# Attention's result reaches the first MLP with the head dimension on partitions, by DMA shifts instead of turns on TensorE

## The reference

```python
# attention: q, k, v are (2, 8, 1152, 64)
q_pool = q.reshape(B, H, S // 2, 2, D).mean(axis=3)              # 576 queries per head
scores = q_pool @ k.T / sqrt(D);  attn = exp(scores - max)
attn = attn / (sum(attn) + 1e-9);  out = attn @ v
x = out.transpose(0, 2, 1, 3).reshape(1152, 512)                 # tokens x (head, head dim)
# first MLP: 512 -> 2048 -> 512
h = x @ w_in;  g = P(h) / (Q(h) + 1e-6);  x = g @ w_out          # P cubic, Q quadratic in |h|
# second MLP: 512 -> 1536 -> 512
xn = x / rms(x) * rms_g;  out = (silu(xn @ w_gate) * (xn @ w_val)) @ w_out2
```

## Time and profile before

| what | value |
|---|---|
| runs of the kernel | 698.08, 700.30 and 1152.23 us; median 700.3 us |
| the profiled execution, by its own time | 701.52 us |
| its span in the trace | 699.7 us |
| PE, PEld (weight loads), DVE, ACT, POOL busy | 98%, 92%, 75%, 60%, 60% of the span |
| attention, first MLP, second MLP | to about 252, to about 457, to the end |

### The profile page before, as it was taken

The page is one execution under the profiler, slowest core; times in us unless marked ns, Lnnn a source line. Parts: engine busy times, 40 slices in busy tenths (PEclk is TensorE's granted clock), DMA queues, the critical chain, the costliest instruction groups (busy, mean ns, idle before and its releaser), DMA issues.

```text
span 699.7 us, 12101 instructions
## 1 busy us (share of the span) xinstructions
PE 686.1 (98%) x4039; PEld 640.5 (92%) x4039; DVE 528.0 (75%) x1026; ACT 420.6 (60%) x874; POOL 417.7 (60%) x417
## 2 busy tenths in 40 slices
PE   8999999999999998899999999999999999999998
PEld 6899999999999998799999998889999999999996
DVE  6889999999999988878898888987654444444432
ACT  5778878888887879777788888954411111111110
POOL 6788878778787576978798788864534430000000
PEclk9999999999999999899999999999999999999999
DMA  8684444634442030101101110113210300000012
GB/s 235 232 216 129 132 132 141 183 114 139 131 122 52 4 119 1 60 1 61 60 17 45 61 61 2 60 61 98 85 60 9 113 1 0 1 1 1 0 61 75
DMA packets 21916, 53.79 MB, mean 77 GB/s; under 512 B 2672, under 2 KB 4784, under 8 KB 21744
## 3 DMA queue, kind: packets, MB, share of 16 engines
q1 hardware_dynamic: 21584, 52.90, 24.5%
q10 hardware_dynamic: 288, 0.33, 0.2%
HBM read 41.42 MB, written 2.36 MB: 63 GB/s over the span
## 4 chain that ended last, share of the span: by engine, by line
PE 87%; POOL 5%; DMA 3%; ACT 2%; issue 1%; SPq 1%; DVE 1%; POOLq 0%; DVEq 0%; ACTq 0%
PE hb L781 30%; PE ob L824 24%; PE sc L667 10%; PE sc L675 8%; PE pv_ps L693 5%; PE misc L693 4%; PE tb L781 3%; DMA qrawA<-in_q 2%; DMA km_lo<-kqB 1%; PE misc L714 1%; POOL num L628 1%; POOL wi_lo L582 1%; PE tb L775 1%; POOL num L626 1%; POOL kqB L520 0%
## 5 line engine op out<-in xcount | busy, mean ns | idle before, releaser
L1069 DVE TENSOR_REDUCE neg_part<-sc 128x1 f32<-128x384 f32 x216 | 108.1, 551 | 12.1 <-PE sc L667 9.9
L894 ACT ACTIVATE pt_hi<-sc 128x384 fp32r<-128x384 f32 x216 | 90.5, 493 | 44.3 <-PE sc L675 44.3
L1080 DVE TENSOR_TENSOR pt_lo<-sc,pt_hi 128x384 fp32r<-128x384 f32 x216 | 106.6, 549 | 2.4 <-ACT pt_hi L894 2.1
L824 PE MATMUL ob<-wo_hi,gt_hi 128*128 128x512 f32 x252 | 100.9, 400 | 4.8 <-DVE gt_lo L1173 2.8
L824 PE MATMUL ob<-wo_lo,gt_hi 128*128 128x512 f32 x252 | 100.6, 399 | 0.0
L824 PE MATMUL ob<-wo_hi,gt_lo 128*128 128x512 f32 x252 | 100.4, 399 | 0.0
L781 PE MATMUL hb<-xt_hi,wi_hi 128*128 128x384 f32 x280 | 95.6, 341 | 0.0
L781 PE MATMUL hb<-xt_lo,wi_hi 128*128 128x384 f32 x280 | 94.4, 337 | 0.0
L781 PE MATMUL hb<-xt_hi,wi_lo 128*128 128x384 f32 x280 | 94.4, 337 | 0.0
L885 ACT ACTIVATE prob<-sc,neg_max 128x1152 f32<-128x1152 f32 x72 | 89.2, 1239 | 3.1 <-DVE neg_max L1073 3.1
L675 PE MATMUL sc<-ident,prob 128*128 128x128 f32 x648 | 82.6, 273 | 0.2 <-ACT prob L885 0.2
(11 more groups left out here) (169 smaller groups left out, 1730.1 us busy)
## 6 DMA issues: line engine op xcount, KB each, us to landing
wraw<-in_moe_w_out SPq DMA_DIRECT2D x7, 1024.0 KB, 5.0
krawB<-in_k SPq DMA_DIRECT2D x8, 576.0 KB, 3.9
qrawB<-in_q SPq DMA_DIRECT2D x8, 512.0 KB, 4.9
wraw<-in_moe_w_in SPq DMA_DIRECT2D x4, 1024.0 KB, 5.2
krawA<-in_k SPq DMA_DIRECT2D x7, 576.0 KB, 5.2
qrawA<-in_q SPq DMA_DIRECT2D x7, 512.0 KB, 6.0
wraw<-in_moe_w_gate SPq DMA_DIRECT2D x3, 1024.0 KB, 4.9
...
```

The costliest lines, as they stand in the source:

```text
L824: ins = nc.tensor.matmul(ob[(m + 1) % 2][:], gt[i][:, f, P * t:P * t + P], wo[c % 2][j][:, f, :], start=f == 0 and n == 0, stop=f == CHUNK ...
L894: nc.scalar.activation(pt[0][:, 3 * c:3 * c + 3, PT_COL[i]:PT_COL[i] + P], src, ACT.Copy).then_inc(pt_hi, 1)
L1069: nc.vector.tensor_reduce(neg_part[:, s, c:c + 1], sc[s][:, c, 0:KBANK], AX.X, ALU.max, negate=True).then_inc(part_done, 1)
L1080: nc.vector.tensor_tensor(pt[1][:, kt, col], src, pt[0][:, kt, col].bitcast(F32), ALU.subtract).then_inc(pt_lo, 1)
```

## The change

`combine`, `divide`, `rows_copy`, `gather`, the turns of tokens for the first MLP and the buffers `o_rows` are gone. Instead SP copies the two halves of `o_sb` to the partitions that the head has in the MLP's input (`shift`, two DMAs inside SBUF), and turns the reciprocals of the row sums into a row that stands on 64 partitions (`rows_of_recip`: DMA to DRAM number by number, a wait, a DMA back that is broadcast). In every second pair POOL sums the halves, scales them and splits them for two heads at once (`sum_parts`, `scale_rows`, `split_x`, 1152 columns each). The last pair goes in pieces: POOL does the columns of groups 0 and 1 (`last_x`), between the splits of the first and the second weights; DVE and ACT do groups 2 and 3 during the first units (`last_scaled`, `last_hi`, `last_lo`). Unit 0 waits for POOL's pieces (`x_lo`); group 3's products stand behind unit 0. `xt` is kept from the start; the buffer `wraw` of raw weights shares its place with attention's, so the first weights are loaded in the last pair. In pair 0 group 0's products move ahead of a scores product, and POOL splits the values ahead of the low queries. POOL's loop over pairs is written out.

```diff
+HALF = KEYS // 2
+
+SUMMED = (0, 5, TILES)
...
+        xt = [sbuf(top, f"xt_{x}", [P, DK, TOKENS], F32R) for x in ("hi", "lo")]
...
-        wraw = sbuf(top, "wraw", [P, DK, CHUNK * P])
...
+            def shift(h, par, n):
+
+                if par == 0:
+                    sp.wait_ge(x_lo, n + 1)
+                sp.wait_ge(o_evac, h * 4 + 4)
+                for e in range(2):
+                    sp.dma_start(o_part[e][64 * par:64 * par + 64, :], o_sb[64 * e:64 * e + 64, :]).then_inc(shifted, 16)
+
+            def rows_of_recip(h, par):
+
+                sp.wait_ge(recip_done, h * 2 + 2)
+                with nc.allow_non_contiguous_dma(reason="one number of each row for each of nine tiles"):
+                    sp.dma_start(recip_rows[par].rearrange("t p -> p t"), recip[:, par]).then_inc(row_out, 16)
+                sp.wait_ge(row_out, h * 16 + 16)
+                sp.dma_start(r_row[64 * par:64 * par + 64, :],
+                             recip_rows[par].rearrange("t p -> (t p)").partition_broadcast(64)).then_inc(row_in, 16)
+
+            def last_rows(n):
+
+                t0, t1 = SUMMED[n], SUMMED[n + 1]
+                sp.wait_ge(recip_done, 2 * PAIRS + 2 * n)
+                with nc.allow_non_contiguous_dma(reason="one number of each row for some tiles"):
+                    sp.dma_start(recip_rows[1, t0:t1].rearrange("t p -> p t"), recip[:, 1, t0:t1]).then_inc(tail_out[n], 16)
+                sp.wait_ge(tail_out[n], 16)
+                sp.dma_start(r_row[64:128, P * t0:P * t1],
+                             recip_rows[1, t0:t1].rearrange("t p -> (t p)").partition_broadcast(64)).then_inc(tail_row[n], 16)
+
+            def last_shift(g):
+
+                sp.wait_ge(o_evac, 4 * PAIRS - 3 + g)
+                col = group_cols(g)
+                for e in range(2 if g < 2 else 1):
+                    sp.dma_start(o_part[e][64:128, col], o_sb[64 * e:64 * e + 64, col]).then_inc(tail_in[g], 16)
+
+            def pair(h, par, n):
+
+                if is_last(h):
+                    mixed_keys(1, h)
+                    load_w(sp, *order[0])
+                    shift(h - 1, 1 - par, n)
+                    rows_of_recip(h - 1, 1 - par)
+                    last_shift(0)
+                    last_rows(0)
+                    last_shift(1)
+                    sp.wait_ge(w_split, 8)
+                    load_w(sp, *order[1])
+                    last_rows(1)
+                    last_shift(2)
+                    last_shift(3)
+                    return
...
-                for x in range(2):
-                    sp.wait_ge(v_split[x], h * 2 + 2)
-                    load_v(x, h + 1)
+                sp.wait_ge(v_split[0], h * 2 + 2)
+                load_v(0, h + 1)
+                if is_first(h):
...
+                else:
+                    shift(h - 1, 1 - par, n)
+                sp.wait_ge(v_split[1], h * 2 + 2)
+                load_v(1, h + 1)
+                if not is_first(h):
+                    rows_of_recip(h - 1, 1 - par)
                 mixed_keys(0, h + 1)
...
+            def sum_parts(h, n):
+
+                pool.wait_ge(k_split[0], h * 2)
+                pool.wait_ge(shifted, n * 64 + 64)
+                nc.gpsimd.tensor_tensor(o_part[0][:], o_part[0][:], o_part[1][:], ALU.add).then_inc(x_sum, 1)
+
+            def scale_rows(n):
+
+                pool.wait_ge(x_sum, n + 1)
+                pool.wait_ge(row_in, n * 32 + 32)
+                nc.gpsimd.tensor_tensor(o_part[0][:], o_part[0][:], r_row[:], ALU.mult).then_inc(x_scaled, 1)
+
+            def split_x(n):
+
+                nc.gpsimd.tensor_scalar(xt[0][:, n], o_part[0][:], 1.0, 0.0, ALU.mult, ALU.add).then_inc(x_hi, 1)
+                pool.wait_ge(x_hi, n + 1)
+                nc.gpsimd.tensor_tensor(xt[1][:, n], o_part[0][:], xt[0][:, n].bitcast(F32), ALU.subtract).then_inc(x_lo, 1)
+
+            def last_x(part, col, n):
+
+                y, d = o_part[0][part, col], DK - 1
+                nc.gpsimd.tensor_tensor(y, y, o_part[1][part, col], ALU.add).then_inc(x_sum, 1)
+                pool.wait_ge(x_sum, n)
+                nc.gpsimd.tensor_tensor(y, y, r_row[part, col], ALU.mult).then_inc(x_scaled, 1)
+                pool.wait_ge(x_scaled, n)
+                nc.gpsimd.tensor_scalar(xt[0][part, d, col], y, 1.0, 0.0, ALU.mult, ALU.add).then_inc(x_hi, 1)
+                pool.wait_ge(x_hi, n)
+                nc.gpsimd.tensor_tensor(xt[1][part, d, col], y, xt[0][part, d, col].bitcast(F32), ALU.subtract).then_inc(x_lo, 1)
+
...
+                if n is not None:
+                    scale_rows(n)
+                    pool.wait_ge(x_scaled, n + 1)
                 mixed_sum(h)
-            def divide(h, par, late):
-
...
-                rows = o_rows[:, 0:TILES - 1]
-                nc.gpsimd.tensor_tensor(rows[:, :, 0:HEAD_DIM], rows[:, :, 0:HEAD_DIM], rows[:, :, HEAD_DIM:], ALU.add).then_inc(rows_sum, 1)
-                pool.wait_ge(rows_sum, h + 1)
-                nc.gpsimd.tensor_tensor(tok[:, :, bass.ds(h * HEAD_DIM, HEAD_DIM)], o_rows[:, :, 0:HEAD_DIM],
-                                        recip[:, par].unsqueeze(2).to_broadcast([P, TILES, HEAD_DIM]), ALU.mult).then_inc(rows_done, 1)
+                if n is not None:
+                    split_x(n)
 
...
-            def pair(h, par):
+            def pair(h, par, n):
                 if is_last(h):
                     pool.wait_ge(k_split[1], h * 2 + 2)
                     values_free(1, h)
                     values_hi(1)
                     values_lo(1, h)
-                    divide(h - 1, 1 - par, False)
-                    for x in range(2):
-                        for f in range(CHUNK):
-                            split_w(order[x], f)
+                    for f in range(CHUNK):
+                        split_w(order[0], f)
+                    pool.wait_ge(w_split, 8)
+                    pool.wait_ge(shifted, 32 * h)
+                    pool.wait_ge(row_in, 16 * h)
+                    last_x(slice(0, 64), slice(HALF, TOKENS), n + 1)
+                    pool.wait_ge(tail_row[0], 16)
+                    for g in range(2):
+                        pool.wait_ge(x_lo, n + 2 + g)
+                        pool.wait_ge(tail_in[g], 32)
+                        last_x(slice(0, P), group_cols(g), n + 2 + g)
+                    for f in range(CHUNK):
+                        split_w(order[1], f)
                 else:
                     split_first_half(h + 1)
-                    if not is_first(h):
-                        divide(h - 1, 1 - par, True)
-                    split_second_half(h + 1)
+                    batch = par == 0 and not is_first(h)
+                    if batch:
+                        sum_parts(h + 1, n)
+                    split_second_half(h + 1, n if batch else None)
 
...
-            def combine(h, part, par):
-
...
-                for n, t in enumerate(PARTS[part]):
-                    ins = nc.tensor.transpose(part_bank(part, par, is_last(h))[:, P * n:P * n + P], o_sb[:, P * t:P * t + P], ident[:])
-                ins.then_inc(comb_t, 1)
-
...
-                    elif i >= 4 or not is_first(h):
+                    elif is_first(h) and i <= 4:
+                        if i >= 3:
+                            pv(0, h, *((0, 8) if i == 3 else (8, 2 * KEY_TILES)))
+                    else:
                         g, j0, j1 = PV_AT[i]
                         pv(g, h, j0, j1)
-                    if i == 2 and not is_first(h):
-                        combine(h - 1, 0, 1 - par)
-                        combine(h - 1, 2, 1 - par)
-                    if i == 3 and not is_first(h):
-                        combine(h - 1, 1, 1 - par)
-                    if i == 7 and is_last(h):
-                        combine(h, 0, par)
-                    if i == 8 and is_last(h):
-                        for t in range(4):
-                            turn_tokens(t, False)
...
-                if f == 0 and c in (0, NC1):
-                    pe.wait_ge(xt_lo, (TILES if mlp2 else 0) + BT * nb + BT)
+                if f == 0 and c == 0:
+                    if nb == 0:
+                        pe.wait_ge(x_lo, PAIRS // 2 + 3)
+                        pe.wait_ge(pt_lo, 27 * PAIRS - 3)
+                    else:
+                        pe.wait_ge(tail_lo, nb)
+                if f == 0 and mlp2 and c == NC1:
...
-            pv(3, PAIRS - 1, 0, 2 * KEY_TILES)
             for u in range(UNITS * NC1):
                 first_product(u)
                 if u == 0:
-                    combine(PAIRS - 1, 1, 1)
-                    combine(PAIRS - 1, 2, 1)
-                for t in TURNED_AT.get(u, ()):
-                    turn_tokens(t, False)
+                    pv(3, PAIRS - 1, 0, 2 * KEY_TILES)
...
-                    act.wait_ge(comb_t, h * 3)
-                nc.scalar.activation(o_sb[:, o0:o0 + n], pv_bank(g, is_last(h) and g == 3)[:, 0:n], ACT.Copy).then_inc(o_evac, 1)
-
...
+            def last_hi(g):
```

(33 more changed lines are left out.)

318 lines of the change are left out of this document (122 added, 196 removed).

## The result

The changed kernel takes 725.0 us (median of four runs, 723.4 to 725.3), the kernel before 699.7 beside it: a ratio of 1.0365 [1.0337, 1.0393]. (One of the four executions of the kernel before took 1152.23 us; the ratio is taken without it.) It is slower by 3.7%, 22 us above the forecast of 703 and outside its range. The profiled run took 725.3, its span is 723.5; the first unit of the MLP stands at 273.25, where the forecast had 253.0.

The account below looks back on a forecast made before the run. PE bounds each pair, POOL with ACT the MLP's first units. None of eleven us of removed PE work arrives; span 699.7 + 2.7 = 702.4, 704.2 against the profiled run, 703 against the median; range 696 to 709.

Parts of the forecast that it names:

- I take 4: SP's queue, each pair: the scatter of 1152 numbers to DRAM takes 4 us, bounds 2.5 and 5.6.
- Behind the scatter's wait stands the copy of the keys `km`, wanted a pair later: nothing: SP's queue in attention: the keys' copy queued behind the scatter's wait costs no time.
- Rival 3: Last pair: SP's two scatters delay POOL's rows once they and SP's issues exceed 12.7 us; 708 us up, chance 0.08.
- Its case of three times the row: Last pair's scatters: writing a 4-byte piece costs three times the reading row, 26.1 us, giving 716 us or more.
- Attention's turns: PE in attention: removing nine turns of `o_sb` from each of seven pairs saves 0.6 us a pair, bounds 0.3 and 0.89.
- The start: First pairs: weights' load leaves the first 20 us, value matmuls fill idle PE, `km_lo` wait goes; gain 1.3 us, bounds 0 and 1.8.
- PE's waits for `v2A` in pairs 3 and 5: First value matmuls of pairs 3, 5 and 7: PE waits 1.53 us because POOL's scaling stands ahead of the values.
- POOL's dependent row as the bound of the first unit: Last pair into MLP: POOL's dependent steps take 35.6 us, first unit starts at 253.0, after a 7.1 us PE wait.
- a clock of 0.50 behind the wait: PE at the MLP's first unit: after about 7 us idle it returns at half speed, 3.84 instead of 1.92 us.
- Pair 3 at 30.23: PE in attention: pairs 3 and 5 near 30.2 us, from 1.53 us of waiting less 0.89 of removed turns.
- The ramp's: MLP's first units: a 5.1 us later start shrinks to a 2.7 us shift at unit 4, which stays; bounds 0 and 5.5.
- The signs named ahead: Trace signs of a wrong forecast: first-unit wait under 3 us or due to a DMA, scatter over 6 us, all pairs alike.

Follow-up runs that it names:

- e4: Changed kernel plus separately waited-for DMA probes in the first MLP; probe g wrote 512 4-byte pieces (7.8 us), another all 1152 (10.9 us); run 756.2 us.
- e9: Changed kernel with each scatter of 4-byte pieces replaced by five serial, waited-for writes of 36-byte runs; 716.1 us, ratio 1.0221 to the kernel before.
- e1: Changed kernel without any scatters or SP's waits for them, rows read from a row of the weights; 700.56 us, ratio 1.0018 to the kernel before.

## Why the prediction was wrong

**The step that failed** is "I take 4" for the scatter of 1152 numbers, with its bounds of 2.5 and 5.6, and with it "Behind the scatter's wait stands the copy of the keys `km`, wanted a pair later: nothing". SP stood 9.0 us at the scatter in its place and 10.9 alone. The bounds came from the one row of 4-byte pieces in the earlier trace rows, but that was a read: 512 pieces from DRAM in 2.5 us. As many written cost 7.8 alone (e4, g). Direction was taken to be of no weight, and both bounds rested on that; the true price lay at 1.6 to 1.9 times the upper one. Nor was `km` wanted a pair later: the copy issued at 130.30 was wanted at 137.85, in the third tile step of the next pair. Rival 3 had the right place, the right chain and the right threshold (12.7 us for two scatters): from the shift at 237.62 to the second broadcast at 263.70 SP took 26.1 us, 13.4 more than that, and POOL's row ended 12.3 late. Its case of three times the row, 26.1 us and 716 us, was closest, yet it stood at a chance of 0.08 because the range of the row was trusted.

**What even rival 3 did not have** is attention. It counts SP's wait in the last pair alone, but SP stands about as long in every pair from 1 on, and behind the wait the copies of `km` go out in one bunch with the broadcast and the next loads. Those of `km_lo` took 7.3 us where they had taken 3.1, and in pairs 4 and 6 PE stood 3.04 and 2.30 us for them, where the prediction had nothing. By e9 the bunch alone makes them late. In pair 4 the copy came 2.3 us later than in e9; 0.9 of that is the longer stand, and where the other 1.4 come from no run shows.

**The sum, step by step.** The first unit came 20.25 us late (273.25 against 253.0): pair 7 began 7.9 late (225.31 against 217.4), and POOL needed 47.9 us from there instead of 35.6, 12.3 more: the two waits for `r_row` are 14.4, and the rest of its row was 2.1 shorter than forecast. Behind the first unit it took 450.2 us, 0.8 more than the forecast's 449.4. Of the 7.9, 5.3 are the waits for `km_lo`. Without scatters (e1) the first two nearly vanish: 218.39, and 34.2 from there.

**Attention's turns** were mis-sized: 0.3 us a pair arrived, not 0.6, the lower bound. DVE shows why, at the maxima of pair 2:

```profile
70.11 1.49 DVE L1109 TENSOR_REDUCE neg_part<-sc 128x1 f32<-128x384 f32 x3 [0.28 <-PE sc L752]
...
89.25 1.49 DVE L1109 TENSOR_REDUCE neg_part<-sc 128x1 f32<-128x384 f32 x3 [0.29 <-PE sc L752]
```

Behind 70.11 DVE's timeline shows no wait until 89.25: through tiles 0 to 4 it is DVE that sets the pace, and the turns stood in tiles 2 and 3. PE had slack there and gets none of it back.

**The start** came nearly as forecast, but not in pair 0. PE's timeline before, then after:

```profile
41.54 1.14 PE L675 MATMUL sc<-ident,prob 128*128 128x128 f32 x9
...
72.06 1.14 PE L675 MATMUL sc<-ident,prob 128*128 128x128 f32 x9
```

```profile
41.43 1.14 PE L760 MATMUL sc<-ident,prob 128*128 128x128 f32 x9
```

Pair 1 begins only 0.1 us earlier. But the wait for `km_lo` of the earlier trace rows, at 50.61, lies in pair 1 and is gone: that pair took 30.52 us and now 70.61 - 41.43 = 29.18, 1.34 less, of which the turns are 0.3. That is 1.1 of the 1.3 us. Pair 0 itself lasts from 29.4 to 34.3 us in the profiled runs here, so its 0.1 says little.

**Right**: PE's waits for `v2A` in pairs 3 and 5, 1.18 and 1.47 us where 1.53 was said; POOL's dependent row as the bound of the first unit (without scatters 252.58, with a PE wait of 4.71 instead of 7.1); a clock of 0.50 behind the wait. Pair 3 at 30.23 where 30.2 was said is partly luck, as both of its terms were smaller: 1.18 for 1.53, and 0.3 for the turns' 0.89.

**The ramp's** 2.7 us are there where they were worked out, but they do not stay. POOL at unit 4 in e1 (272.39 in the earlier trace rows), and the busy time of e1 in the stretch that answers to the second of the earlier trace rows:

```profile
275.29 1.00 POOL L706 TENSOR_TENSOR num<-num,h 128x384 f32<-128x384 f32 x1 [3.97 <-ACT lin L995]
```

```profile
276.00:300.00 24.00, 20.17 (x98) 17.71 (x99) 20.66 (x36) 20.55 (x43) 23.12 (x23) 1.00 0.13 44
```

Unit 4 is 2.9 us later than before; at unit 15 POOL is 0.3 us later (318.77 and 318.43). Before, the clock fell to 0.50 in that stretch, with a mean of 0.87; in e1 it is 1.00. The forecast took the work behind the ramp to last as long as before. From the first unit to the end e1 took 698.2 - 252.58 = 445.6 us, the kernel before 447.8 by the earlier trace rows. In sum e1's span of 698.2 is 4.2 under the forecast's 702.4: 1.0 later at pair 7, 1.4 shorter in POOL's row, 3.8 shorter behind the first unit.

**The signs named ahead** read rightly: "a scatter landing in over 6 us" and waits "put down to a DMA (`r_row`)" are what the trace shows.
